# A second mixture of experts that takes its tokens in the order of the first one's slots

## The chip, the core and the metric

The kernel runs on one core of a Trainium2 chip. The core has TensorE (PE in the profile, its weight loads PEld), VectorE (DVE), ScalarE (ACT), GpSimd (POOL) and SyncE (SP), which only issues transfers here. The metric is the device time of one execution in microseconds, the median of several runs.

## The reference

Attention with pooled queries (2 batches, 8 heads, 1152 keys, 576 queries, 64 features) gives 1152 tokens of 512 features. Two mixtures of 8 experts each (hidden size 1024) follow. The first sends each token to one expert and drops what exceeds a capacity of 288 slots:

```python
expert_idx = np.argmax(x @ w_gate, axis=1)
gate_w = probs[np.arange(N), expert_idx]            # softmax of the logits
for i in range(N):                                  # slots in the order of tokens
    e = expert_idx[i]
    if counts[e] < capacity:
        disp[e, counts[e]] = x[i]; pos[i] = counts[e]; counts[e] += 1; keep[i] = True
h = np.maximum(np.einsum('ecd,edf->ecf', disp, w1), 0.0)
y = np.einsum('ecf,efd->ecd', h, w2)
out[i] = gate_w[i] * y[expert_idx[i], pos[i]]       # where keep[i], else 0
```

The second lets every expert work on every token and adds them with weights P, which come from the exponential of the logits (less their overall maximum) by eight rounds of scaling its rows and its columns:

```python
for e in range(E):
    out += P[:, e:e + 1] * (np.maximum(x @ w1[e], 0.0) @ w2[e])
```

P needs sums over all tokens, but no order of them. A dropped token enters the second mixture as zeros.

## The kernel before

Each engine has its own program, written out by hand, and they meet in semaphores. There is no scheduler: an engine does its instructions in the order of its program, and a queue its transfers in the order of issue. Products are done in three passes of split numbers (a high part, and a residue that is the value less the high part): `L1240` hidden products, `L1253` and `L1272` output products. ScalarE makes the high parts from PSUM, VectorE the residues; for weights ScalarE makes the high parts (`L512`), POOL the residues (`L448`, `L453`).

Attention: 16 heads (`head` on each engine), each of five tiles of queries. In tile t, TensorE turns the probabilities of tile t (`L1107`) and makes the scores of tile t+2 (`L1097`), into four buffers `prob`; in tile 3 it also turns out the head before (`L1140`). POOL's `split_head(g)` splits the keys, queries and values of a head that SP has loaded, L424 first and L440 last. Ahead of head 4's loads SP fills `slots_in` with zeros (L338), and one row of `slots_out` (L340).

Routing: each batch of eight heads is routed by itself, the first within heads 9 to 11, the second behind head 15. VectorE finds the best expert (L820 to L834), TensorE counts with triangular ones (`prefix`), VectorE makes the slot `sidx` (L840 to L854) and, for the way back, `gidx` (L859 to L862), and POOL scatters the rows of `x` to `slots_in` by `sidx` (L461). The gate's weight is worked out last (L908 to L922).

First mixture (`expert1`): ScalarE loads an expert's 288 rows from `slots_in`, TensorE turns them in four chunks of 128 features (`turn_rows`, L1228) within the expert before. Eight blocks of hidden products go through four PSUM banks, then four groups of 24 output products (`project_t`, L1272), one per chunk of 128 features, leave the results transposed: features on partitions, tokens along columns. ScalarE copies each (L633), TensorE turns it back into rows (`turn_back`, L1285), VectorE copies it out (L941), ScalarE stores the rows to `slots_out`. Experts 1 to 6 are a loop at run time on every engine.

Between the mixtures: POOL gathers the rows of each tile of tokens by `gidx` (L496), VectorE multiplies them by the gate (L972), TensorE turns them (`turn_tile`, L1199), ScalarE and VectorE split them into `xts`. The first three tiles come before the first hidden product, the other seven beside the next ones.

Second mixture (`expert2`): per expert three groups of 384 tokens, each of 8 x 12 hidden products and 3 x 24 output products; VectorE adds them into `acc` (L1064). The first expert also makes the logits and P (`gate_columns`, L1207, and `first_steps`). At the end ScalarE stores each tile of `acc` to the output as soon as it is done (L707).

## Time and profile before

| | |
|---|---|
| Median of 3 runs | 1359.14 us (1358.27 to 1360.24) |
| The profiled execution | 1359.23 us |
| Its span | 1357.5 us |
| Busy in the span | PE 97%, PEld 90%, DVE 39%, ACT 37%, POOL 36% |
| L1240 hidden products, both mixtures | 3072, 518.2 us busy |
| L1253, second mixture's output products | 1728, 397.7 us |
| L1272, first mixture's output products | 768, 114.1 us |
| L1285, results turned back | 96, 15.7 us |
| L1199, gathered tiles turned | 40, 7.4 us |

Busy time tells which engine is full and hardly where a change counts: matmuls are pipelined, and their ends are modelled. The chain that ended last is followed back from the last instruction, at each step to what released it; its pieces are on the path. A timeline row has start, length, engine, source line, operation, output and inputs, the number of instructions merged (x3), and in brackets the idle time of the engine ahead of it and what ended that. "issue" is time for which the profile shows no cause. SPq and ACTq rows are the issuing of transfers.

### The profile page before, as it was taken

How to read it: one execution, taken by the hardware profiler on the slowest of the kernel's cores; microseconds unless marked ns; L12 is line 12 of the kernel's file. 1: busy time of each engine (PE TensorE's matmuls, PEld its weight loads, DVE VectorE, ACT ScalarE, POOL GpSimd, SP SyncE). 2: the span in 40 equal slices, each digit the busy share in tenths (PEclk: the TensorE clock that was granted, in tenths of full speed). 3: DMA queues.
4: the chain of work that ended last, by engine and by line, in shares of the span. 5: the costliest groups of instructions: out<-in, count | busy, mean ns of one | idle time of the engine just before them, and what ended most of it. 6: DMA issues, size and time to landing. Idle time of an engine off the chain costs nothing.

```text
span 1357.5 us, 21723 instructions
## 1 busy us (share of the span) xinstructions
PE 1311.1 (97%) x7814; PEld 1225.4 (90%) x7814; DVE 522.7 (39%) x1326; ACT 505.0 (37%) x1032; POOL 488.9 (36%) x405
## 2 busy tenths in 40 slices
PE   6999999959999996999999999999999999999998
PEld 6999989949999996898999999999999999999998
DVE  7999999942222222326311112211112211112211
ACT  6777777745554553212212212212212213113111
POOL 6555556348775777102303203203203203204100
PEclk9999999979999998999999999999999999999999
DMA  4722223137666555201201201201101101100001
GB/s 134 228 96 101 97 77 112 52 135 243 205 207 189 161 183 176 89 1 32 94 0 32 93 0 52 72 0 62 62 0 62 62 0 62 62 0 0 0 0 70
DMA packets 60861, 111.95 MB, mean 82 GB/s; under 512 B 5215, under 2 KB 15779, under 8 KB 60808
## 3 DMA queue, kind: packets, MB, share of 16 engines
q1 hardware_dynamic: 52488, 94.63, 21.4%
q10 hardware_dynamic: 6848, 12.09, 2.7%
q0 software_dynamic: 1472, 4.54, 1.0%
q8 instruction: 31, 0.51, 0.2%
q14 instruction: 22, 0.18, 0.0%
HBM read 97.27 MB, written 14.16 MB: 82 GB/s over the span
## 4 chain that ended last, share of the span: by engine, by line
PE 92%; DVE 4%; issue 2%; DMA 1%; ACT 1%; POOL 0%; ACTq 0%; DVEq 0%; POOLq 0%
PE psum L1240 37%; PE psum L1253 29%; PE psum L1272 7%; PE psum L1097 6%; PE psum L1107 5%; PE psum L1122 5%; PE psum L1140 1%; PE psum L1285 1%; PE psum L1228 1%; DVE small L723 1%; DVE acts L732 1%; DVE raw L723 1%; DMA raw<-in_k_dram 0%; PE psum L1207 0%; ACT wsplit L512 0%
## 5 line engine op out<-in xcount | busy, mean ns | idle before, releaser
L1240 PE MATMUL psum<-acts,wsplit 128*128 128x384 f32 (+1 forms) x3072 | 518.2, 328 | 1.5 <-issue 1.5
L1240 PEld LDWEIGHTS psum<-acts,wsplit 128*128 128x128 f32 x3072 | 508.3, 190 | 3.8 <-issue 2.0
L1253 PE MATMUL psum<-wsplit,acts 128*128 128x512 f32 x1728 | 397.7, 390 | 0.0
L1253 PEld LDWEIGHTS psum<-wsplit,acts 128*128 128x128 f32 x1728 | 323.7, 188 | 66.3
L448 POOL TENSOR_TENSOR wsplit<-raw,wsplit 128x512 fp32r<-128x512 f32 x128 | 162.5, 1296 | 497.7 <-ACT wsplit L512 497.7
L626 ACT ACTIVATE acts<-psum 128x384 fp32r<-128x384 f32 (+1 forms) x256 | 120.7, 471 | 570.9 <-PE psum L1240 570.3
L932 DVE SCALAR_TENSOR_TENSOR acts<-psum,acts 128x384 fp32r<-128x384 f32 (+1 forms) x256 | 136.1, 532 | 374.9 <-ACT acts L626 374.7
L453 POOL TENSOR_TENSOR wsplit<-raw,wsplit 128x512 fp32r<-128x512 f32 x128 | 161.1, 1297 | 130.2 <-ACT wsplit L512 130.1
L512 ACT ACTIVATE wsplit<-raw 128x512 fp32r<-128x512 f32 (+1 forms) x259 | 155.7, 623 | 87.1 <-PE psum L1253 75.2
L1064 DVE SCALAR_TENSOR_TENSOR x<-psum,pr,x 128x512 f32<-128x512 f32 x63 | 47.3, 751 | 293.5 <-PE psum L1253 293.5
L512 ACT ACTIVATE acts<-psum 128x384 fp32r<-128x384 f32 (+2 forms) x282 | 117.1, 457 | 75.1 <-PE psum L1107 46.2
L732 DVE TENSOR_TENSOR acts<-psum,acts 128x384 fp32r<-128x384 f32 (+1 forms) x240 | 122.1, 510 | 7.0 <-ACT acts L512 6.4
L1272 PE MATMUL psum<-acts,wsplit 128*128 128x288 f32 x768 | 114.1, 300 | 0.0
L1097 PE MATMUL psum<-wsplit,acts 128*128 128x384 f32 x480 | 105.7, 356 | 7.4 <-DVE acts L873 7.4
L1272 PEld LDWEIGHTS psum<-acts,wsplit 128*128 128x128 f32 x768 | 103.1, 188 | 0.0
L1122 PE MATMUL psum<-acts,wsplit 128*128 128x256 f32 (+1 forms) x576 | 90.4, 297 | 0.6 <-ACT small L535 0.6
L1097 PEld LDWEIGHTS psum<-wsplit,acts 128*128 128x128 f32 x480 | 82.2, 193 | 7.5 <-issue 7.4
L1122 PEld LDWEIGHTS psum<-acts,wsplit 128*128 128x128 f32 x576 | 83.3, 188 | 0.7 <-DVE acts L732 0.7
L424 POOL TENSOR_TENSOR small<-small 128x576 f32<-128x576 f32 x15 | 21.3, 1419 | 94.2 <-PE psum L1097 74.5
L1107 PE MATMUL psum<-ident,small 128*128 128x128 f32 x360 | 49.1, 275 | 5.5 <-DVE acts L732 4.4
L519 ACT ACTIVATE small<-small,low 128x1152 f32<-128x1152 f32 x40 | 50.5, 1261 | 2.1 <-DVE small L723 2.1
L1107 PE MATMUL psum<-ident,raw 128*128 128x128 f32 x360 | 49.4, 278 | 1.8 <-DVE acts L732 1.4
(128 smaller groups left out, 728.3 us busy)
## 6 DMA issues: line engine op xcount, KB each, us to landing
raw<-in_moe_w_dram SPq DMA_DIRECT2D x64, 1024.0 KB, 5.1
raw<-in_k_dram SPq DMA_DIRECT2D x15, 576.0 KB, 5.9
small<-in_q_dram SPq DMA_DIRECT2D x15, 576.0 KB, 3.9
small<-in_v_dram SPq DMA_DIRECT2D x16, 288.0 KB, 4.3
slots_in<-zero SPq DMA_DIRECT2D x1, 4608.0 KB
small<-slots_in ACTq DMA_DIRECT2D x7, 576.0 KB, 4.7
slots_out<-small ACTq DMA_DIRECT2D x7, 576.0 KB, 7.1
out_dram<-x ACTq DMA_DIRECT2D x9, 256.0 KB, 2.4
```

The costliest lines, as they stand in the source:

```text
L448: pool.tensor_tensor(w1s[1][:, :, fs], raw1[hf][:, :, rsl], w1s[0][:, :, fs].bitcast(F32), ALU.subtract).then_inc(lo_done, 1)
L453: pool.tensor_tensor(w2s[1][:, f, :], raw2[f // (FC // 2)][:, f % (FC // 2), :], w2s[0][:, f, :].bitcast(F32), ALU.subtract).then_inc(lo_d ...
L512: nc.scalar.activation(out, in_, ACT.Copy).then_inc(s, 1)
L626: nc.scalar.activation(hs[0][:, f, 0:w], psum[:, f % HBANKS, 0:w], ACT.Relu).then_inc(h_hi, 1)
L732: nc.vector.tensor_tensor(pts[r][1][:, js, col:col + qw(t)], psum[:, BPT + m % TBANKS, 0:CH].rearrange("p (j n) -> p j n", j=JC)[:, :, 0:q ...
L932: nc.vector.scalar_tensor_tensor(hs[1][:, f, 0:w], psum[:, f % HBANKS, 0:w], 0.0, hs[0][:, f, 0:w].bitcast(F32), ALU.max, ALU.subtract).th ...
L1097: last = mm(psum[:, s_bank(t, c), 0:CH], qs[u][i][:, t * P:(t + 1) * P], ksp[u][:, c * CH:(c + 1) * CH], start=(i == 0), stop=(i == 1))
L1107: last = nc.tensor.transpose(psum[:, BPT + m % TBANKS, j * P:(j + 1) * P], prob[buf(v, t)][:, (c * JC + j) * P:(c * JC + j + 1) * P], iden ...
L1122: last = mm(psum[:, BPV, 0:GW[r]], vsp[v % 2][:, j, :], pts[r][i][:, j, :], start=(n == 0), stop=(n == VSTEPS - 1))
L1240: last = mm(psum[:, f % HBANKS, 0:w], w1s[a][:, c, f * P:(f + 1) * P], src[z][:, c, cols], start=(i == 0), stop=(i == 3 * DC - 1))
L1253: last = mm(psum[:, bank, :], hs[a][:, f, t0:t0 + P], w2s[z][:, f, :], start=(i == 0), stop=(i == 3 * FC - 1))
L1272: last = mm(psum[:, BY + c % 2, 0:CAP], w2s[a][:, f, c * P:(c + 1) * P], hs[z][:, f, 0:CAP], start=(i == 0), stop=(i == 3 * FC - 1))
```

## The change

The results of the first mixture stay on the chip, transposed as they come, and the second mixture takes the tokens in the order of experts and slots instead of their own.

- The gate's weight multiplies the rows before they are scattered. It is positive, and the maximum with zero keeps it. VectorE works it out within the routing (`gate_input`, `gate_weight`); rows of batch 0 are scaled by POOL in heads 11 to 13, those of batch 1 by ScalarE (two tiles) and VectorE (three).
- TensorE adds up how many tokens each expert has (`totals`), VectorE makes of it at which column each expert's tokens start (`expert_starts`), and the token's place (`owner_index`). POOL scatters each token's number to `owners` by it, within experts 0 to 3.
- `y_cols` on ScalarE and VectorE splits the four groups of an expert's results straight into `xts`, from the starting column on, which each engine reads into a register once per expert (`value_load`). Columns behind an expert's last token are written over by the next expert; ScalarE clears those past the last (`clear_x`).
- The first four hidden blocks of the second mixture begin with three of their four chunks of features.
- SP clears the output ahead of head 4's loads, since dropped tokens have no owner; POOL scatters the tiles of `acc` to the output by `owner`.
- For room: three probability buffers, values in another place, `xts` 288 columns wider, `dts` apart from it. The experts of the first mixture are written out on all engines, in place of a loop.

The diff, cut:

```diff
-        NP = 4
+        NP = 3
...
+            sp.dma_start(out.rearrange("(p a) (b c) -> p (a b) c", p=P, c=P),
+                         zero[:, :].unsqueeze(1).broadcast_to([P, NT * DC, P])).then_inc(out_cleared, 16)
+            sp.wait_ge(consts, 20)
+            sp.dma_start(owners.rearrange("(p a) o -> p (a o)", p=P), nobody[:, :]).then_inc(owners_cleared, 16)
...
+            def scale_early(t):
+                pool.wait_ge(x_done, NH)
+                pool.wait_ge(gate_done, 1)
+                part = x[0:qw(t), t, 0:DM]
+                pool.tensor_tensor(part, part, gate[0:qw(t), t:t + 1].broadcast_to([qw(t), DM]),
+                                   ALU.mult).then_inc(scaled0, 1)
...
+            def own(n):
+                w = qw(n % QT)
+                pool.indirect_dma_start(
+                    out=owners, out_offset=bass.IndirectOffsetOnAxis(ap=cidx[0:w, n:n + 1], axis=0),
+                    in_=token[0:w, n:n + 1], in_offset=None,
+                    bounds_check=N - 1, oob_is_err=False).then_inc(owned, 16)
...
+                if n == 1:
+                    pool.wait_ge(cidx_done, 1)
+                    pool.wait_ge(owners_cleared, 16)
+                for m in OWN.get(n, ()):
+                    own(m)
...
+            pool.wait_ge(owner_loaded, 16)
+            pool.wait_ge(out_cleared, 16)
+            for n in range(NT):
+                pool.wait_ge(y_done, NT * (E - 1) + n + 1)
+                pool.indirect_dma_start(
+                    out=out, out_offset=bass.IndirectOffsetOnAxis(ap=owner[:, n:n + 1], axis=0),
+                    in_=acc[:, n, :], in_offset=None,
...
+            def y_cols(e, start_e, c):
+                if e:
+                    act.wait_ge(yx_done, DC * (e - 1) + c + 1)
+                split_hi(xts[0][:, c, bass.ds(start_e, CAP)], psum[:, BY + (DC * e + c) % 3, 0:CAP], yx_hi)
...
+                if e == 0:
+                    act.wait_ge(starts_ready, 1)
+                start_e = act.value_load(starts[0:1, e:e + 1], min_val=0, max_val=min(e * CAP, N))
+                if e:
+                    act.wait_ge(x_cleared, 2 * min(e, N // CAP - 1))
...
+            def gate_weight(b):
+                ts = tiles(b)
+                dve.wait_ge(ex_done, b + 1)
+                rstep(nc.vector.tensor_reduce(sume[:, ts], ex[:, ts, :], AXX, ALU.add))
+                rstep(nc.vector.tensor_scalar_add(sume[:, ts], sume[:, ts], EPS))
+                nc.vector.reciprocal(gate[:, ts], sume[:, ts]).then_inc(gate_done, 1)
...
             one_hot(1)
+            gate_input(1)
             scale_output(G - 1)
+            gate_weight(1)
             slot_limit(1)
             slot_number(1)
             scatter_index(1)
...
+            for t in range(ACT_ROWS, QT):
+                scale_rows(t)
+            expert_starts()
+            owner_index()
...
+            def y_cols(e, start_e, c):
+                if c == 0 and e:
+                    dve.wait_ge(x_cleared, 2 * min(e, N // CAP - 1))
+                dve.wait_ge(yx_hi, DC * e + c + 1)
+                cols = bass.ds(start_e, CAP)
+                nc.vector.tensor_tensor(xts[1][:, c, cols], psum[:, BY + (DC * e + c) % 3, 0:CAP],
+                                        xts[0][:, c, cols].bitcast(F32), ALU.subtract).then_inc(yx_done, 1)
...
+                if DC * e + c >= 3:
+                    pe.wait_ge(yx_done, DC * e + c - 2)
...
+                    opening = HBANKS if first and g == 0 else 0
+                    for f in range(opening):
+                        pe.wait_ge(h_done, FC * E + f - HBANKS + 1)
+                        hidden(E, f, xts, cols, TG, range(DC - 1), yx_done if f == 0 else None, DC * (E - 1))
+                    for f in range(opening):
+                        hidden(E, f, xts, cols, TG, range(DC - 1, DC), yx_done if f == 0 else None, DC * (E - 1))
+                    for f in range(opening, FC):
+                        pe.wait_ge(h_done, FC * E + NG * FC * e + FC * g + f - HBANKS + 1)
+                        hidden(E + e, f, xts, cols, TG, range(DC), None, 0)
```

In the instructions TensorE's stream changes at the seam of the mixtures. Before, from the middle of the last expert's last output group on (L1285 turns results back, L1199 turns gathered tokens, L1240 is the second mixture's first hidden block):

```order
L1272 MATMUL psum<-acts,wsplit 128x288 x12
L1285 MATMUL psum<-ident,small 96x128 [waits y_done,yt_done]
L1285 MATMUL psum<-ident,small 96x128 x2
L1199 MATMUL psum<-ident,x 128x128 [waits x2_scaled]
L1199 MATMUL psum<-ident,x 128x128 x3
L1199 MATMUL psum<-ident,x 128x128 [waits x2_scaled]
L1199 MATMUL psum<-ident,x 128x128 x3
L1199 MATMUL psum<-ident,x 128x128 [waits x2_scaled]
L1199 MATMUL psum<-ident,x 128x128 x3
L1240 MATMUL psum<-acts,wsplit 128x384 [waits lo_done,xt_done,h_done]
L1240 MATMUL psum<-acts,wsplit 128x384 x11
```

and afterwards (L1311 is the output group, L1279 a hidden block):

```order
L1311 MATMUL psum<-acts,wsplit 128x288 [waits yx_done]
L1311 MATMUL psum<-acts,wsplit 128x288 x23
L1279 MATMUL psum<-acts,wsplit 128x384 [waits yx_done,lo_done,h_done]
L1279 MATMUL psum<-acts,wsplit 128x384 x2
L1279 MATMUL psum<-acts,wsplit 128x384 [waits yx_done]
L1279 MATMUL psum<-acts,wsplit 128x384 x2
L1279 MATMUL psum<-acts,wsplit 128x384 [waits yx_done]
L1279 MATMUL psum<-acts,wsplit 128x384 x2
L1279 MATMUL psum<-acts,wsplit 128x384 [waits lo_done,h_done]
L1279 MATMUL psum<-acts,wsplit 128x384 x8
L1279 MATMUL psum<-acts,wsplit 128x384 [waits lo_done,h_done]
L1279 MATMUL psum<-acts,wsplit 128x384 x8
```

The transposes are gone, and so is the wait for gathered rows; the last chunk's columns are waited for only where the fourth chunk begins, further on.

VectorE behind the choice of the second batch's experts, before (`oh` marks the expert, `sidx` is the slot):

```order
L834 TENSOR_TENSOR oh<-eqr,st 128x40 [waits route_step]
L761 TENSOR_TENSOR x<-psum,den 128x5x64
L840 TENSOR_TENSOR cnt<-elim,oh 128x40 [waits oh_done]
L841 TENSOR_REDUCE st<-cnt 128x5 [waits route_step]
L847 TENSOR_TENSOR cnt<-psum,oh 128x40 [waits pos_ready,route_step]
L849 TENSOR_REDUCE st<-cnt 128x5 [waits pos_read]
L853 TENSOR_TENSOR st<-st 128x5 [waits route_step]
L854 SCALAR_TENSOR_TENSOR sidx<-st 128x5 [waits route_step]
L859 SCALAR_TENSOR_TENSOR st<-st 128x5
L861 TENSOR_SCALAR st<-st 128x5 [waits route_step]
L862 CAST gidx<-st 128x5 [waits route_step]
```

and afterwards (L906 is the exponential's input, L911 to L913 the gate's weight in `st`, L887 the limit):

```order
L882 TENSOR_TENSOR oh<-eqr,st 128x40 [waits route_step]
L906 TENSOR_TENSOR tmp<-lg,st 128x40
L810 TENSOR_TENSOR x<-psum,den 128x5x64
L911 TENSOR_REDUCE st<-ex 128x5 [waits ex_done]
L912 TENSOR_SCALAR st<-st 128x5 [waits route_step]
L913 RECIPROCAL st<-st 128x5 [waits route_step]
L887 TENSOR_SCALAR st<-st 128x5
L894 TENSOR_TENSOR cnt<-psum,oh 128x40 [waits pos_ready,route_step]
L896 TENSOR_REDUCE st<-cnt 128x5 [waits pos_read]
L900 TENSOR_TENSOR st<-st 128x5 [waits route_step]
L901 SCALAR_TENSOR_TENSOR sidx<-st 128x5 [waits route_step]
L920 TENSOR_SCALAR x<-x,st 128x512 [waits x_done,gate_done]
```

Three operations of the gate now stand ahead of the slot, one more ahead of the scaling of the output, and the three for `gidx` are gone.

ScalarE in an expert of the loop, where its hidden evacuations end, before (L621 and L630 prepare the waits of the loop, L512 writing `acts` splits turned tokens, L633 takes a result):

```order
L512 ACTIVATE wsplit<-raw 128x4x128
L625 REGISTER_ALU
L626 ACTIVATE acts<-psum 128x288 [waits h_ready]
L512 ACTIVATE wsplit<-raw 128x4x128
L621 REGISTER_ALU
L512 ACTIVATE acts<-psum 128x288 [waits dt_ready]
L621 REGISTER_ALU
L512 ACTIVATE acts<-psum 128x288 [waits dt_ready]
L630 REGISTER_ALU
L632 REGISTER_ALU [waits y_ready]
L633 ACTIVATE small<-psum 128x288 [waits rows_ready]
```

and afterwards (L713 reads the register; L564 writing `acts` with `yx_done` splits a result):

```order
L686 ACTIVATE acts<-psum 128x288 [waits h_ready]
L564 ACTIVATE wsplit<-raw 128x4x128
L713 TENSOR_LOAD starts
L713 ISA x2
L564 ACTIVATE acts<-psum 128x288 [waits dt_ready,x_cleared]
L564 ACTIVATE acts<-psum 128x288 [waits dt_ready]
L564 ISA [waits yx_done,y_ready]
L564 ACTIVATE acts<-psum 128x288
```

The register load stands between the last weight split and the first turned tokens of the next expert.

## Rows read from the trace of the kernel before

**Rows 1.** Page, chain that ended last: shares of the span by engine.

```profile
PE 92%; DVE 4%; issue 2%; DMA 1%; ACT 1%; POOL 0%; ACTq 0%; DVEq 0%; POOLq 0%
```

**Rows 2.** Chain, one expert of mixture one: start us, us, what it consists of.

```profile
361.18 1.58 PE psum L1240 x12
...
380.02 0.33 PE psum L1285 x3
...
389.17 1.59 PE psum L1240 x12
```

**Rows 3.** Timeline, TensorE between the mixtures: start us, us, engine line op out<-in xcount [idle<-releaser].

```profile
526.16 1.82 PE L1272 MATMUL psum<-acts,wsplit 128*128 128x288 f32 x12
...
537.23 1.12 PE L1199 MATMUL psum<-ident,x 128*128 128x128 f32 x4 [7.61 <-DVE x L972]
...
542.57 4.18 PE L1240 MATMUL psum<-acts,wsplit 128*128 128x384 f32 x12 [1.46 <-issue]
```

**Rows 4.** Chain, second mixture, first and a steady stretch.

```profile
565.81 5.48 PE psum L1253 x24
...
660.47 16.66 PE psum L1240 x96
```

**Rows 5.** Timeline between the mixtures, ScalarE's last result and POOL's first gather.

```profile
528.65 0.39 ACT L633 ACTIVATE small<-psum 128x288 f32<-128x288 f32 x1
...
533.10 1.07 POOL L496 DMA_INDIRECT x<-slots_out,gidx  x1 [1.20 <-DMA slots_out<-small]
```

**Rows 6.** Timeline, routing of the second batch.

```profile
287.80 0.19 DVE L840 TENSOR_TENSOR cnt<-elim,oh 128x40 f32<-128x40 f32 x1
...
288.91 0.17 DVE L854 SCALAR_TENSOR_TENSOR sidx<-st 128x5 uint32<-128x5 f32 x1
...
289.88 1.01 POOL L461 DMA_INDIRECT slots_in<-x,sidx  x1 [31.46 <-DVE gidx L862]
...
290.04 0.23 DVE L920 TENSOR_REDUCE st<-ex 128x10 f32<-128x80 f32 x1 [0.34 <-ACT ex L604]
```

**Rows 7.** Chain, the scatter of the second batch.

```profile
293.74 0.97 POOL slots_in L461
...
295.02 2.31 DMA slots_in<-x,sidx
```

**Rows 8.** Timeline, where an expert's hidden products end: ScalarE and TensorE's weight loads.

```profile
374.62 0.62 ACT L512 ACTIVATE wsplit<-raw 128x512 fp32r<-128x512 f32 x1
...
376.09 0.28 PEld L1228 LDWEIGHTS psum<-ident,small 96*128 96x128 f32 x3 [0.18 <-DVE acts L926]
```

**Rows 9.** Timelines of SP, POOL and TensorE around heads 4 and 5.

```profile
35.94 15.63 SPq L340 DMA_DIRECT2D slots_out<-zero  x1
...
59.38 1.41 POOL L424 TENSOR_TENSOR small<-small 128x576 f32<-128x576 f32 x1 [10.64 <-DMA small<-in_q_dram]
...
67.52 1.41 POOL L440 TENSOR_TENSOR acts<-small,acts 128x576 fp32r<-128x576 f32 x1
...
75.34 1.29 PE L1097 MATMUL psum<-wsplit,acts 128*128 128x384 f32 x6
...
91.79 0.42 PE L1097 MATMUL psum<-wsplit,acts 128*128 128x384 f32 x1
```

**Rows 10.** Windows: length, busy PE, PEld, DVE, ACT, POOL, clock, DMA share, GB/s.

```profile
40.00:44.00 4.00, 4.00 (x34) 3.97 (x34) 3.94 (x11) 2.56 (x6) 3.83 (x4) 1.00 1.12 334
232.00:248.00 16.00, 15.93 (x120) 15.49 (x119) 15.21 (x48) 12.52 (x28) 9.67 (x9) 1.00 0.21 65
```

**Rows 11.** Timeline of head 9, POOL beside VectorE.

```profile
181.26 1.42 POOL L440 TENSOR_TENSOR acts<-small,acts 128x576 fp32r<-128x576 f32 x1
...
181.63 1.11 DVE L840 TENSOR_TENSOR cnt<-elim,oh 128x40 f32<-128x40 f32 x1
```

**Rows 12.** Timeline, POOL's w2 residues, with the idle time ahead.

```profile
386.83 6.31 POOL L453 TENSOR_TENSOR wsplit<-raw,wsplit 128x512 fp32r<-128x512 f32 x5 [7.93 <-ACT wsplit L512]
```

**Rows 13.** Timeline, VectorE's last accumulation.

```profile
1354.27 0.75 DVE L1064 SCALAR_TENSOR_TENSOR x<-psum,pr,x 128x512 f32<-128x512 f32 x1 [4.68 <-PE psum L1253]
```

433 lines of the change are left out of this document (194 added, 239 removed).

## The prediction, made before the changed kernel ran

> **What bounds the kernel now.** I read the shares of the chain that ended last first, then the chain row by row where the change acts, then the timelines around those places. The chain lies on TensorE for 92% of the span [rows 1]: what counts is how many microseconds TensorE multiplies, transposes or waits. Three places matter.
>
> In the first mixture an expert takes 28.0 us (361.18 to 389.17) [rows 2]. In it stand the products, the transposes of the next expert's tokens, and four transposes of finished results back into rows, each 0.33 us on the chain [rows 2].
>
> Between the mixtures TensorE's last product starts at 526.16 and twelve products of 288 columns take 1.6 (0.134 us each, the 12 behind 361.18 take 1.58), so it ends at 527.75 [rows 2, 3]. The first transpose of gathered tokens follows at 537.23, the first hidden product at 542.57 [rows 3], and the first output product at 565.81 [rows 4]. POOL's first gather starts only at 533.10, after the stored rows have landed [rows 5]. In the steady state the 96 hidden products between those two points take 16.66 [rows 4].
>
> Behind the attention, the routing of the second batch goes through a string of short VectorE operations that ends at 289.08, then POOL scatters [rows 6]; nothing else runs on TensorE there.
>
> **What the change takes away.**
> 1. Transposes back. Experts 0 to 7 have 4 each; the last of expert 7 stands behind the final product, and expert 0 has three within its stream, as the rest of its four stands in expert 1. That makes 31 within the stream, 31 x 0.33 = 10.2 us, all on the chain. The copies and stores that followed them lay beside products. The work put in their place is one ScalarE and one VectorE operation per 128 features, as before, and the output ring of three banks instead of two lets TensorE do two further groups of 24 products (3.2 us each) before it must wait for either. Term: -10.2.
> 2. The hand-over. From the last product to the first output product of the second mixture it is 565.81 - 527.75 = 38.1 us. Afterwards the 96 hidden products follow at once: 16.7. Its cover: the first 36 of them (four banks, three of the four feature chunks) take 36 x 0.174 = 6.2 us, until 534.0 on the old scale, and need nothing of the last chunk. ScalarE took up that last chunk at 528.65 [rows 5] behind seven weight splits, and VectorE follows within about 1 us: 4 us to spare. The banks come free in time too: the four are finished 0.52 apart, bank 0 is asked for again 1.56 after its end, and its two evacuations take about 1. Term: 38.1 - 16.7 = -21.4.
>
> **What it adds or moves.**
> 3. The gate in the routing. The weight must be in the rows before they are scattered. Order on VectorE: one operation ahead of the scaling of the output, three behind it, and one less for the limit. The sum behind the exponential waited 0.34 for ScalarE [rows 6]; the output's scaling, which now stands between, covers that. Three linked operations of 0.17 to 0.23 and one of 0.2, less one of 0.2: sidx comes 0.7 later than 289.08. Scaling two tiles on ScalarE and three on VectorE (at most 0.62 each, as a weight split [rows 8]) lies beside POOL, whose scatters stand 1.28 apart [rows 7]. ScalarE's weight splits now begin behind it, at some 290.2; 12 of at most 0.62 end at 297.6, ahead of the scatter's landing at 297.3 + 0.7 [rows 7]. Past that each would delay the load of the rows. Term: +0.7 (bounds 0.2 and 1.5).
> 4. Clearing the output. 4608 more pieces of 512 B (2.36 MB) stand in SP's queue right in front of head 4's keys and queries. SP sat 15.63 us at the small copy behind the 4.72 MB zero fill before it gave out head 4's loads; POOL began its split of them at 59.38, after waiting 10.64 for the queries, and its last operation ended at 68.93. TensorE's scores of head 4 began at 75.34: 6.4 us of slack. The queues carried 334 GB/s then, of which the fill is about 305 (4.72 MB in 15.5): 2.36 MB are 7.7 us [rows 9, 10]. Head 4 is ready at 76.6, 1.3 late. Head 5's queries, asked for when POOL is done, land some 4 us later, and POOL's 9.55 us of work ends near 90.3, before TensorE asks for it (91.79 + 1.3). VectorE is busy 3.94 of 4 us there [rows 10], so nothing wins this back. Term: +1.3 (bounds 0 and 3: below if only part of the fill's time goes ahead of the load, above if head 5 is caught as well).
> 5. Reading the expert's first column. On ScalarE a register load stands between the last hidden evacuation with its weight split and the evacuation of the next expert's first turned tokens; TensorE waits for the latter already, 0.18 us each time [rows 8]. The trace has no such load. Lower bound 0: the weight split before it starts at 374.62 and takes 0.62, and a load given out beside it is hidden. Upper bound 1.3: the distance from one POOL scatter to the next, the only instructions here that read an index in memory [rows 7]. I take 0.3, near the lower end since 0.5 of the engine's own time can hide it; seven experts have a successor: +2.1 (bounds 0 and 9.1). VectorE's load hides the same way.
> 6. Heads 9 to 13. VectorE loses 1.11 at 181.63 for an operation that takes 0.19 at 287.80 when POOL is still [rows 6, 11]. A single-operand form replaces it in the same place, four short operations are added in heads 9 and 10, three leave head 11, and POOL scales five tiles (1.3 each, by its splits of the same size [rows 12]) in heads 11 to 13, where VectorE's reciprocals run. Added and removed nearly balance. Term: +0.5 (bounds -1 and 2).
> 7. The end. The last accumulation ends at 1355.02, and with ScalarE's store the span of 1357.5 ends 2.5 later [rows 13]. POOL instead starts 0.8 to 0.9 after its release (289.08 to 289.88, [rows 6]) and its scatter lands 2.3 after the start [rows 7]. Term: +0.8 (bounds -0.2 and 1.9).
> 8. At nothing: three probability buffers (the wait for the third-last tile's turning is implied by TensorE's own order of scores), the other place of the values, clearing of columns on ScalarE (1152 elements, 1.4 by the 0.62 of 512, twice in three experts; a step of 1.6 us uses some 1.0 of it, and there are four banks), the owners' scatters (three of 1.3 in POOL's idle 7.93 before the w2 residues [rows 12]; uncovered they would be 13 us of weights), their load, and the straight-line experts.
>
> **Two rules weighed.** Rows 8 show what follows the place of the register load, not the load. The Trainium skill, Runtime: NRT & Kernel Launch, under Instruction fetch mechanics, has about 200 ns per register for such a load, and under The ~15µs preamble/postamble breakdown 1.3 us for several words from HBM. As an estimate, the first makes seven loads 1.4 and hidden, the second 9.1 and mostly seen. No run here shows it for SBUF.
>
> Rows 11 show VectorE's 1.11 ending (182.74) as POOL's operation ends (182.68). The Trainium skill, SBUF — State Buffer, under Who interferes with whom, says that a VectorE operation with two SBUF inputs and a GpSimd operation that reads SBUF shut each other out for a whole instruction. By that rule, the trace agrees, POOL's new scaling speaks against the change: up to 1.3 per head for three heads, the upper bound of step 6 and more.
>
> **The sum.** 1359.23 - 10.2 - 21.4 + 0.7 + 1.3 + 2.1 + 0.5 + 0.8 = 1333.0 us. The profiled execution's 1359.23 (span 1357.5 and 1.7 around it) lies 0.1 above the median of the runs, so this stands for the median too.
>
> **The rivals.**
> A. The register load waits until ScalarE is drained. For: it must follow its engine's order, and TensorE waits at that spot already. Against: 0.5 of cover. Price 1.3 x 7 = 9.1 in place of 2.1: 1340.0.
> B. The attention gives back more: head 5 caught too, POOL's scaling in VectorE's way in three heads. For: VectorE is busy 15.21 of 16 us. Against: POOL is busy 9.67 of 16 [rows 10]. Price 1.7 (step 4's upper bound) + 1.5 (step 6's) + 2 beyond it: about 1338.
> C. Steps 4 to 6 are hidden. For: 6.4 of slack and 0.5 of cover are of the order of the costs. Price -3.9: 1329.1.
> D. Slower: the first mixture's experts, now straight code with twice the instructions before the second mixture, starve TensorE of instructions. It decides from (26.2 + 2.7) / 8 = 3.6 us per expert on; at 4 us each the time is 1333.0 + 32 = 1365. Against: the heads are straight code already, and the two windows of rows 10 show TensorE busy 4.00 of 4 and 15.93 of 16 us.
> E. The change does not do what it says: the second mixture still waits, since the last chunk comes behind the weight splits. From 4 us lateness on; to keep even 10 of the 21.4 (time 1343) the last chunk would need to be 14 late. Against: rows 5.
>
> **Chances.** Forecast 0.55 (1330 to 1336.5), A 0.16, B 0.1, C 0.14, D 0.02, E 0.03. The range to hold 8 in 10 takes in C and most of A and B: 1328 to 1341. Differences under 0.2% (2.7 us) can't be told from none here; faster 0.97, the same 0.01, slower 0.02: only D ends there.
>
> **What would show it.** Steps 1 and 2: no transposes but those of tokens in an expert, about 26.7 us plus the load's share per expert, and the output product of the second mixture some 17 us behind the last of the first, with no idle TensorE between. Step 4: head 4's scores wait about 1.3 for POOL. Step 5: TensorE's wait before the second transpose of an expert, 0.18 now, is 0.5; at 1.5 it is A. Step 3: the first scatter 0.7 later against the end of the attention. Step 7: 3.2 from the last accumulation to the end. Wrong would be an expert over 28 us, an idle TensorE between the mixtures, or a gap above 3 us at head 4 or 5.

## The result, and the profile after

| | before | after |
|---|---|---|
| median of 4 runs each, us | 1359.69 (1358.27 to 1362.77) | 1341.51 (1340.81 to 1342.95) |
| ratio, 95% interval | | 0.987 (0.9858 to 0.9883) |
| profiled execution, span | 1359.23, 1357.5 | 1340.81, 1339.1 |
| TensorE busy | 1311.1 | 1296.7 |

The changed kernel is faster by 1.3%. The forecast was 1333.0, with 1341 as the range's end: the direction and the large terms were right, but 7.8 us of the 26.2 forecast did not come, and the result lies outside the range. Spans divided at the same events show where:

| stretch | before | after | difference | forecast |
|---|---|---|---|---|
| start to turning out head 15 | 284.45 | 289.39 | +4.9 | +1.8 (steps 4, 6) |
| to the second batch's first scatter | 5.43 | 5.76 | +0.3 | +0.7 (step 3) |
| to expert 0's first hidden product | 13.11 | 13.31 | +0.2 | 0 |
| to the end of mixture one's last product | 224.76 | 217.36 | -7.4 | -8.1 (steps 1, 5) |
| to mixture two's first output product | 38.06 | 16.85 | -21.2 | -21.4 (step 2) |
| to TensorE's end | 788.24 | 790.65 | +2.4 | 0 |
| to the end of the span | 3.45 | 5.78 | +2.3 | +0.8 (step 7) |

The page's chain by engine answers to [rows 1]: still TensorE, one point less.

```profile
PE 91%; DVE 3%; issue 1%; ACT 1%; DMA 1%; POOL 1%; POOLq 0%; DVEq 0%; ACTq 0%
```

The chain through one expert of mixture one (start us, us, what), against [rows 2]: 365.72 to 392.62 is 26.90 in place of the 27.99 between 361.18 and 389.17, and no transpose is left but those of tokens (L1268). The issue of 0.03 at 380.39 is all that shows where the register load stands. In [rows 8] the second transpose's weight load waited 0.18.

```profile
365.72 12.80 PE psum L1279 x96
378.52 0.25 PE psum L1268 x3
378.76 1.62 PE psum L1311 x12
380.39 0.03 issue
380.42 0.44 PE psum L1268 x3
...
382.73 3.23 PE psum L1311 x24
...
392.62 2.40 PE psum L1279 x18
```

The chain between the mixtures, against [rows 3, 4]: the hidden products follow the last output products with no gap, and at 542.67 the first output products follow them.

```profile
513.02 12.80 PE psum L1311 x96
525.82 16.84 PE psum L1279 x96
```

The steady stretch of mixture two, against [rows 4]: 96 hidden products take 16.84 where they took 16.66, and nothing waits.

```profile
653.23 16.34 PE psum L1292 x72
669.57 16.84 PE psum L1279 x96
```

The timelines of the queue of SyncE, of POOL and of TensorE at heads 3 and 4, against [rows 9] (three cuts of three timelines). SyncE gives out head 4's keys at 59.64 (before: 51.61), behind two clearings that hold its queue. POOL starts on them 8.3 late. What TensorE lacks is not head 4's scores, as forecast, but the values of head 3, which POOL splits in the same round (L441, ends at 75.11): it idles 4.42.

```profile
35.75 16.38 SPq L357 DMA_DIRECT2D out_dram<-zero  x1
52.17 7.42 SPq L360 DMA_DIRECT2D owners<-nobody  x1
59.64 1.20 SPq L320 DMA_DIRECT2D raw<-in_k_dram  x1
...
67.72 1.43 POOL L453 TENSOR_TENSOR small<-small 128x576 f32<-128x576 f32 x1 [19.82 <-DMA small<-in_q_dram]
...
73.71 1.40 POOL L441 TENSOR_TENSOR wsplit<-raw,wsplit 128x576 fp32r<-128x576 f32 x1
...
69.49 1.29 PE L1139 MATMUL psum<-wsplit,acts 128*128 128x384 f32 x6
75.21 2.05 PE L1164 MATMUL psum<-acts,wsplit 128*128 128x256 f32 x8 [4.42 <-issue]
77.05 2.12 PE L1149 MATMUL psum<-ident,small 128*128 128x128 f32 x9
...
80.89 1.27 PE L1182 MATMUL psum<-raw,small 128*128 128x72 f32 x10
```

The same two points before, the product with head 3's values and the turning out of head 2, which stands in head 3:

```profile
73.28 1.10 PE L1122 MATMUL psum<-acts,wsplit 128*128 128x256 f32 x8
...
76.47 1.23 PE L1140 MATMUL psum<-raw,small 128*128 128x72 f32 x10
```

Behind the gap everything is slow: nine transposes in 2.12, where nine took 1.14 at 68.59. The windows (columns as in [rows 10]) show why: behind the idle time the granted clock is at 0.50, 1.2 in place of 2.4 GHz.

```profile
70.00:75.00 5.00, 0.79 (x5) 0.47 (x3) 2.80 (x9) 1.67 (x4) 4.75 (x4) 0.91 0.00 0
75.00:78.00 3.00, 2.79 (x13) 2.82 (x14) 0.00 (x0) 0.07 (x1) 2.13 (x3) 0.50 0.00 0
78.00:82.00 4.00, 4.00 (x23) 4.00 (x21) 2.61 (x8) 2.64 (x5) 0.66 (x1) 0.63 0.95 303
```

The chain in expert 0: it comes from the landing of late weights, and TensorE stands idle for 1.19 ahead of the second transposes (row with e8 below).

```profile
311.09 10.30 DMA raw<-in_moe_w_dram
```

The end, against [rows 13]: the timeline's last addition ends at 1334.30, the scatter's record starts at 1335.09 and the span ends at 1339.1.

```profile
1333.54 0.75 DVE L1106 SCALAR_TENSOR_TENSOR x<-psum,pr,x 128x512 f32<-128x512 f32 x1 [4.68 <-PE psum L1292]
1335.09 0.97 POOL L555 DMA_INDIRECT out_dram<-x,owner  x1 [4.46 <-DVE x L1106]
```

### The profile page after: what moved, and what is told of

The parts are those of the page before. It is cut to its first block, busy times and chain, and to the rows that moved or that the text cites. A ratio compares the mean times of both kernels' runs of the same rounds, so it can differ in the third digit from the quotient of the medians.

```text
span 1339.1 us, 20887 instructions
## 1 busy us (share of the span) xinstructions
PE 1296.7 (97%) x7688; PEld 1213.4 (91%) x7688; DVE 508.0 (38%) x1313; ACT 505.7 (38%) x1031; POOL 502.9 (38%) x423
## 4 chain that ended last, share of the span: by engine, by line
PE 91%; DVE 3%; issue 1%; ACT 1%; DMA 1%; POOL 1%; POOLq 0%; DVEq 0%; ACTq 0%
PE psum L1279 36%; PE psum L1292 29%; PE psum L1311 8%; PE psum L1149 6%; PE psum L1139 5%; PE psum L1164 5%; PE psum L1182 1%; DMA raw<-in_moe_w_dram 1%; POOL wsplit L479 1%; DVE raw L772 1%; PE psum L1268 1%; DVE acts L781 1%; DVE small L772 0%; ACT acts L564 0%; ACT raw L571 0%
## 5 line engine op out<-in xcount | busy, mean ns | idle before, releaser
L1279 PE MATMUL psum<-acts,wsplit 128*128 128x384 f32 (+1 forms) x3072 | 515.4, 328 | 0.0
L1279 PEld LDWEIGHTS psum<-acts,wsplit 128*128 128x128 f32 x3072 | 509.3, 189 | 1.8
L564 ACT ACTIVATE wsplit<-raw 128x512 fp32r<-128x512 f32 (+1 forms) x259 | 155.3, 623 | 85.2 <-PE psum L1292 75.0
L564 ACT ACTIVATE acts<-psum 128x384 fp32r<-128x384 f32 (+2 forms) x304 | 123.1, 448 | 121.4 <-PE psum L1311 55.5
L1311 PE MATMUL psum<-acts,wsplit 128*128 128x288 f32 x768 | 109.2, 298 | 0.0
L1311 PEld LDWEIGHTS psum<-acts,wsplit 128*128 128x128 f32 x768 | 103.2, 188 | 0.0
L1149 PE MATMUL psum<-ident,raw 128*128 128x128 f32 x477 | 64.4, 275 | 4.1 <-ACT raw L571 2.2
L571 ACT ACTIVATE raw<-raw,low 128x1152 f32<-128x1152 f32 x53 | 66.9, 1262 | 0.0
L772 DVE TENSOR_SCALAR_CACHE_REDUCE raw<-psum,low 128x384 f32<-128x384 f32 x106 | 64.4, 607 | 0.1
L1149 PEld LDWEIGHTS psum<-ident,raw 128*128 128x128 f32 x477 | 52.7, 140 | 10.6 <-ACT raw L571 5.2
```

The lines of the kernel that those rows point to most:

```text
L564: nc.scalar.activation(out, in_, ACT.Copy).then_inc(s, 1)
L1149: last = nc.tensor.transpose(psum[:, BPT + m % TBANKS, j * P:(j + 1) * P], prob[buf(v, t)][:, (c * JC + j) * P:(c * JC + j + 1) * P], iden ...
L1279: last = mm(psum[:, f % HBANKS, 0:w], w1s[a][:, c, f * P:(f + 1) * P], src[z][:, c, cols], start=(c == 0 and (a, z) == (0, 0)), stop=(c == ...
L1311: last = mm(psum[:, BY + (DC * e + c) % 3, 0:CAP], w2s[a][:, f, c * P:(c + 1) * P], hd[z][:, f, :], start=(i == 0), stop=(i == 3 * FC - 1))
```

## The experiments

All are edits of the changed kernel (1341.5, ratio 0.987) but e4, an edit of the kernel before. Ratios are to the kernel before as it ran beside each group of them (medians 1358.4 to 1360.2 us), with 95% intervals. A single letter is the theory of that name in the expectation above it. Code is cut, with "..." for what is left out.

| | median, us | ratio |
|---|---|---|
| e1_pitch1408 | 1336.84 | 0.9831 (0.9811 to 0.9851) |
| e2_late_clear | 1334.95 | 0.9831 (0.9812 to 0.985) |
| e3_vector_clears | 1351.4 | 0.9944 (0.9927 to 0.996) |
| e4_before_odd | 1363.25 | 1.0031 (1.002 to 1.0042) |
| e5_shift | 1336.94 | 0.9837 (0.9824 to 0.9851) |
| e6_fixed_starts | 1340.03 | 0.9858 (0.9843 to 0.9873) |
| e7_direct_store | 1338.36 | 0.9837 (0.9824 to 0.9851) |
| e8_clears_later | 1340.27 | 0.9855 (0.9838 to 0.9872) |
| e9_owners_late | 1341.15 | 0.9855 (0.984 to 0.987) |
| e10_no_opening | 1343.13 | 0.9874 (0.9859 to 0.989) |
| e11_pitches | 1335.8 | 0.9825 (0.9811 to 0.9838) |
| e12_all | 1329.5 | 0.9769 (0.9756 to 0.9783) |
| e13_pitch1344 | 1337.59 | 0.9841 (0.9816 to 0.9866) |
| e14_hold | 1343.99 | 0.9892 (0.9874 to 0.991) |

### The fill: e2 and e9

e2 issues the output's clearing far later, behind the loads of the second mixture's first expert, and the owners' behind those of head 6:

```diff
-sp.dma_start(out..., zero...).then_inc(out_cleared, 16)      # ahead of head 4
+sp.dma_start(out..., zero...).then_inc(out_cleared, 16)      # behind load_expert(1, 0, E)
```

> The changed kernel with the clearing of the output moved in SP's queue from ahead of head 4's loads to behind the loads of the second mixture's first expert, and the small clearing of owners to behind head 6's loads. Theory F (fill): the fill alone held head 4's queries back 8.3 us, TensorE idled 4.4 at head 3 and then ran some 5 us at half the granted clock, and head 4 lost 1.1 to a POOL that was shifted. The turning-out behind head 15 then goes from 289.39 to about 283.1, time 1335.2. Rival G (gate work): POOL's scaling of rows and the gate's operations in heads 9 to 13 take part of the 4.9; then it stays above 285. Rival H: with the fill away the old stall at head 2 (2.1 us, VectorE's 1.8 us operation beside POOL) returns in full on top: time 1337.

Head 15 was turned out at 283.45, 5.9 earlier, and the time fell by 6.6: F. In its timeline POOL starts on head 4 at 58.97 and TensorE has no gap at the values of head 3. H's old stall did come back (TensorE idles 0.93 and 0.55 for VectorE ahead of 68.12, where the kernel before idled 0.90 and 0.55), within the 5.9 and not on top of them. G is out: 283.45 is under its 285, and ahead of the kernel before.

```profile
35.73 16.47 SPq L320 DMA_DIRECT2D raw<-in_k_dram  x1
...
72.87 1.11 PE L1165 MATMUL psum<-acts,wsplit 128*128 128x256 f32 x8
```

e9 tells which clearing is to blame; it moves the owners' alone.

> Only the filling of the small table of owners (7.42 us in SyncE's queue in the changed kernel, 52.17 to 59.59) goes behind head 6's loads; the clearing of the output stays ahead of head 4. Head 4's keys are then issued at 52.2 and not at 59.64 (before: 51.61). O, the owners' table is what makes head 4 late: no 4.42-us wait of TensorE at head 3, turning out behind head 15 begins at 283.5 to 284.5 and not at 289.39, time about 1336. Q, the 16 us of clearing ahead of it keep the loads late by filling the DMA engines, wherever the table's issue stands: 288 to 289, 1341.

```profile
35.57 16.27 SPq L357 DMA_DIRECT2D out_dram<-zero  x1
51.89 7.55 SPq L320 DMA_DIRECT2D raw<-in_k_dram  x1
...
74.74 1.61 PE L1165 MATMUL psum<-acts,wsplit 128*128 128x256 f32 x8 [4.31 <-issue]
```

The 7.5 us simply went over to head 4's keys, which now stand in that place, and head 15 was turned out at 287.84: Q, though not quite as written. The row's time is not that of its own transfer. Whatever stands first behind the 4.7-MB fill sits 15.6 to 16.5 us in SyncE's queue (slots_out of 2 KB before, the output's clearing after, the keys in e2), and what stands behind the 2.4-MB clearing sits 7.4 to 7.6. A small DMA carries the wait for its predecessors in the profile.

### The distance between rows: e1, e4, e5, e13, e11

The change made a row chunk of xts 1440 columns (5760 B) long in place of 1152 (4608 B). e1 takes 1408 (5632 B), e4 gives the kernel before 1184 (4736 B), with hd at 288 and dts at 384.

```diff
-        XW = N + CAP
+        XW = 1408
```

> The changed kernel with one difference: a chunk of the second mixture's tokens (xts) lies 1408 columns behind the last instead of 1440, 5632 B = 11 x 512 B instead of 5760 B = 22.5 x 256 B. Theory P (pitch): TensorE reads its moving columns more slowly where a chunk does not begin on a round address; the 96 hidden products of the second mixture go back from 16.84 us to the 16.66 of the kernel before, in 24 groups: 24 x 0.18 = 4.3 us, time 1337.2. Rival L (load): the 0.18 comes from what else changed around them (clock, other engines at SBUF); 16.84 stays, time 1341.5.

> The kernel before with three pitches changed and nothing else: xts 1184 columns (4736 B, no multiple of 256) in place of 1152, the first mixture's hidden values 288 columns in place of 384, its turned tokens 384 in place of 288. Theory P: three separate readings: hidden products of the second mixture 16.66 -> 16.84 per 96, output products of the first 3.16 -> 3.21 per 24, hidden products of the first 12.80 -> 12.65 per 96; in sum 4.3 + 1.6 - 1.1 = +4.8 us, time 1364. Rival L: all three as before, 1359.4.

Both fit P. e4 shows its other two readings as well: in mixture one 96 hidden products take 1.58 + 11.06 = 12.64, where the kernel before took 1.58 + 11.19, and an expert's output products some 0.1 more. From the chains, e1 first, then e4, each in the steady stretch of mixture two:

```profile
669.94 16.66 PE psum L1279 x96
```

```profile
660.14 16.84 PE psum L1244 x96
```

From mixture two's first hidden product to the last scatter e1 takes 2.6 us less (1332.25 - 525.38 against 1335.09 - 525.66), not the 24 x 0.18 = 4.3 of the hidden products: the output products take 16.36 for 16.34, and in e1 the clock dropped once more, in the gate's steps (12 products in 3.16 for 2.31, the next 24 in 4.77 for 4.22; see the last section). e5 shifts both halves by 256 B at distance 1408:

> Row distance of xts 1408 columns as in e1, but both halves begin 64 columns (256 B) further on, so that every stretch that the hidden products read begins 256 B off the place it had. In e1 96 hidden products took 16.66 us, in the changed kernel (where chunks 1 and 3 of 4 lie 256 B off and 0 and 2 do not) 16.84. P, the distance between the rows is what counts: 16.66 us, and 806.9 us from the first hidden product of mixture two to the last scatter, as in e1 (about 1337). A, the place of each read counts, and half of them are misplaced in the changed kernel: all are now, 16.66 + 2 x 0.18 = 17.02 us, 24 groups make 8.6 us more, 815.5 (about 1346).

It has 16.66 too (at 667.62), so A is out: not where a stretch begins but how far apart the rows are. e13 tells which distances:

> Row distance of xts 1344 columns, 5376 B: a multiple of 256 B (21) and not of 512 B (10.5). The slow distances so far (5760, 4736 and 1152 B) are multiples of neither, the fast ones (4608, 5632 and 1536 B) of both. H, whole 512 B are needed: 96 hidden products of mixture two in 16.84 us, about 1341. Q, whole 256 B do: 16.66 us, about 1338.

```profile
669.44 16.66 PE psum L1279 x96
```

Q: 5376 B, 21 x 256, is fast. All fast distances tried are whole multiples of 256 B, the slow ones are not. e11 gives hd and dts whole multiples as well (1536 B for 1152):

```diff
-        XW = N + CAP
-        HD = 2 * FC * CAP
+        XW = 1152
+        HD = 2 * FC * TG
...
-        hd = [acts[...FC * CAP...] ...]
+        hd = [hs[i][:, :, 0:CAP] for i in (0, 1)]
+        dts = ... DC * TG ... [:, :, 0:CAP]
```

> All operands that TensorE reads as columns lie in rows whose distance is a multiple of 512 B: xts 1152 columns (4608 B; these inputs' slots end at column 1114), hd and dts 384 (1536 B). R, the distance is what made the products slower: 96 hidden products of mixture two 16.66 us for 16.84 (24 groups, less 0.02 for each of 24 output groups: 2.4 us in all as measured with 1408), the period of an expert 26.90 less 0.24 (output products 12 in 1.58 for 1.61) and less 0.14 (hidden products 96 in 12.66 for 12.80, as with the distance 384 in the kernel before): 8 x 0.38 = 3.0 us; 1336.1. V, only xts matters: 1339.1.

R, but less than its 3.0 us: the expert's period is 26.64 (the chain below), so 8 x 0.26 = 2.1. The hidden products are as expected (12.64), the output products of mixture one went only from 3.23 to 3.19 per 24. The hidden part was not lost by the change: dts lay at 1152 B in the kernel before too. The change moved hd alone in mixture one, from 1536 B to 1152.

```profile
363.71 12.64 PE psum L1279 x96
...
380.56 3.19 PE psum L1311 x24
...
390.35 9.74 PE psum L1279 x74
```

### The clears of slots: e3 and e8

e3 lets VectorE make the clears of columns, with the same shape:

```diff
-                nc.scalar.activation(xts[i][:, :, k * CAP:(k + 1) * CAP], zero..., ACT.Copy)
+                nc.vector.tensor_copy(xts[i][:, :, k * CAP:(k + 1) * CAP], zero...)
```

> The changed kernel with the six clearings of columns done by VectorE instead of ScalarE, at the same places. Theory C (clears): in expert 0 ScalarE comes late to the first turned tokens because of two clearings of 1.17 us, and TensorE waits 1.19 us for them; without them the wait is about 0.2, time 1340.4. Rival W (weights): ScalarE is late there because expert 1's first weights land late (it waits 4.39 and 0.66 for them in expert 0); the wait stays at 1 or more and the time at 1341.5.

All theories missed: 10 us slower than the changed kernel. The timelines of VectorE, POOL and TensorE in expert 0:

```profile
318.38 12.30 DVE L1003 CAST acts<-zero 128x1152 fp32r<-128x1152 f32 x1
...
331.34 0.80 DVE L1003 CAST acts<-zero 128x1152 fp32r<-128x1152 f32 x1
...
320.16 9.90 POOL L479 TENSOR_TENSOR wsplit<-raw,wsplit 128x512 fp32r<-128x512 f32 x8
...
333.37 0.71 PE L1267 MATMUL psum<-ident,x 96*128 96x96 f32 x3 [9.12 <-DVE acts L984]
```

A copy that takes 0.80 when POOL splits nothing took 12.30 and ended at 330.68, 0.6 us behind POOL's row of splits (330.06). ScalarE's clear of the same shape takes 1.17 beside the same splits. It is the effect that [rows 11] show at 1.11 for 0.19, but here VectorE did not get in between POOL's operations and waited for the rest of the row, about nine of them. That is one of the six clears. The other four that ran beside such a row, in experts 1 and 2, took 1.44, 1.28, 1.44 and 1.27, and they did get in between: POOL's own split beside them took 1.83 for 1.3.

```profile
354.77 1.44 DVE L1003 CAST acts<-zero 128x1152 fp32r<-128x1152 f32 x1
...
355.54 1.83 POOL L479 TENSOR_TENSOR wsplit<-raw,wsplit 128x512 fp32r<-128x512 f32 x1
```

What made the first one wait so long stays open. The Trainium skill, SBUF — State Buffer, under Who interferes with whom, has copies and casts of VectorE that use both port pairs shut out GpSimd and be shut out by it for whole instructions, and ScalarE wait for no one; by that page this was the engine not to move the clears to, and the trace agrees. In expert 0 TensorE idled 9.12, 7.9 more than in the changed kernel, and behind it the granted clock was at 0.50 (window 333:336); together that is most of the 10 us.

e8 moves expert 0's two clears by ScalarE into expert 1. It does one thing more than its expectation says: the clears that experts 1 and 2 have of their own come one step later (`f in (4, 6)` in place of `(3, 5)`).

> The two clears of slots that ScalarE makes in expert 0 (1.17 and 1.15 us) are made in expert 1 in front of its own two, where ScalarE is idle half of the time; nothing else moves. S, the clears are what makes ScalarE late in expert 0: the one behind the last late weight (322.76) lies on the chain, the first lies in a wait for that weight, so 1.05 us of the 1.19 us in front of L1268 go, 1340.4. W, the late weights alone do it: 1.19 us stay, 1341.5. B, four clears in expert 1 hold up the hidden splits: a new wait of TensorE there of up to 2 us, 1343.

The profiled span is that of the changed kernel, 1339.1. The timelines of ScalarE, VectorE and TensorE in expert 0, the changed kernel first:

```profile
321.42 0.63 ACT L564 ACTIVATE wsplit<-raw 128x512 fp32r<-128x512 f32 x1 [0.66 <-DMA raw<-in_moe_w_dram]
...
326.60 0.44 PE L1268 MATMUL psum<-ident,x 96*128 96x96 f32 x3 [1.19 <-DVE acts L991]
```

```profile
322.32 0.63 ACT L564 ACTIVATE wsplit<-raw 128x512 fp32r<-128x512 f32 x1 [2.22 <-DMA raw<-in_moe_w_dram]
...
325.85 0.46 DVE L993 TENSOR_TENSOR acts<-psum,acts 128x288 fp32r<-128x288 f32 x1 [0.46 <-ACT acts L564]
...
326.46 0.44 PE L1270 MATMUL psum<-ident,x 96*128 96x96 f32 x3 [0.81 <-POOL wsplit L479]
```

From the split of the late weight to the second transposes it is 5.18 in the changed kernel and 4.14 in e8. The other runs repeat it: 5.15 to 5.19 in the ten that leave ScalarE's clears where they were, 4.13 in e12, which moves them. So 1.04 us of expert 0's wait are the second clear's, which stands behind that split, as S has it. They did not show in full in e8's wait, 0.81 for 1.19, because the weight itself landed 0.9 later there. POOL, which the profile names as what ended the wait, is a coincidence: the transposes wait for VectorE's residue (`dt_done`), which ended at 326.31, and POOL's operation ended at 326.36.

What e8 gained it gave back in experts 1 and 2. There the later clear holds the next transposes, 0.33 of idle TensorE each where 0.03 to 0.05 stood. In expert 2, whose chain follows, that can only come from the shift of its own clears, since none of expert 0's stands there.

```profile
378.01 0.96 ACT acts L696
...
380.82 0.44 PE psum L1270 x3
```

With the clears in place the wait in expert 0 is anything from 0.47 (e6) to 1.81 (e1), mostly according to when that weight lands against TensorE's products.

### The register load: e6

```diff
-                start_e = act.value_load(starts[0:1, e:e + 1], ...)
+                start_e = min(144 * e, N - CAP)
```

The kernel leaves out the experts' own first columns, so its output is not the reference's.

> The experts' first columns are constants, 144 x e, and nothing is loaded into registers; the second mixture's columns are then not the experts' own slots, and its output is not the reference's. T, the trace of the changed kernel is right that the load costs 0.06 us in each of 7 experts: 0.4 us less, 1341.1, the expert's period stays 26.90 less 0.06, and the 0.24 us in front of L1268 becomes 0.18. P, the prediction's 0.3 us an expert: 2.1 us less, 1339.4. A, the register load drains its queue: 9 us less, 1332.4.

The time fell by 1.5, and the ratios' intervals overlap. The trace is clearer: hidden blocks start at 417.66 and 444.58, a period of 26.92 as with the load (419.52 and 446.41: 26.89), and the place of the load shows 0.05 of issue (378.49). What this execution gained lies in the fill (288.35) and in expert 0's wait. The load costs nothing that can be seen, less even than T's 0.06; P and A are out.

### The end: e7

```diff
-                pool.indirect_dma_start(out=out, out_offset=...owner..., in_=acc[:, n, :], ...)
+                act.dma_start(out[n * P:(n + 1) * P, :], acc[:, n, :])
```

The kernel leaves out the way back to the tokens' own rows.

> The ten output tiles are stored by ScalarE's direct DMAs in the order of slots in place of GpSimd's scatter by owner, so the output's rows are not in the reference's order. In the changed kernel the last scatter is issued at 1335.09 behind 0.51 + 1.19 us of queue on GpSimd and the span ends 4.0 us later, 4.76 us behind the last addition (1334.33); before, the span ended 3.45 us behind TensorE's last product, now 5.78. E, the indirect scatter is what makes the end longer: 2.3 us less, 1339.2. N, a direct store's landing takes as long: 1.7 us of queue less at most on GpSimd and as much back on ScalarE, 1341 or more.

```profile
1334.14 0.75 DVE L1105 SCALAR_TENSOR_TENSOR x<-psum,pr,x 128x512 f32<-128x512 f32 x1 [4.68 <-PE psum L1291]
1334.92 0.34 ACTq L756 DMA_DIRECT2D out_dram<-x  x1
```

The span ends at 1337.3, 2.4 behind the addition's end (1334.89), for 4.8 with the scatter: E.

### The hand-over: e10 and e14

e10 drops the opening (`opening = 0`); e14, whose edit is shown, keeps it and makes its first product wait for the fourth column group.

```diff
+                    if opening:
+                        pe.wait_ge(yx_done, DC * E)
```

> The second mixture's first hidden products no longer begin with the three column groups that are ready and come back for the fourth; the first of them waits until the last expert's fourth group is split. In the changed kernel they begin at 525.82 and VectorE's last split is 527.35 + 0.46 and 0.14 to TensorE. M, the opening is what closes the hand-over without idle time: TensorE waits 2.1 us before its first product, 1343.6. N, something else (the order of the weights) holds the first products anyway: no wait, 1341.5. C, the clock falls behind the wait as it does at head 3: 2.1 us and up to 3 us more, 1346.

> TensorE waits for the last expert's fourth column group before the first hidden product of mixture two; the products keep their new order. In e10 only the fourth chunk's products waited (0.46 us), since three chunks of the first column group, 1.6 us of products, still ran ahead. M, the late group is covered by the 36 products ahead of it and by nothing else: TensorE idles 2.1 us from 525.8 on (527.35 + 0.46 + 0.14), 1343.6, and its clock stays whole. C, the clock falls behind this gap as behind the 4.42 us at head 3: 2.5 us more, 1346. N, the group is there sooner than VectorE's record shows: under 1 us, 1342.

e10's time is close to M's 1343.6, but not for M's reason. Its timeline shows 0.46 of idle and not 2.1, since nine products of the first block still ran ahead, and the granted clock stayed at 1.00 (window 528:532). From its first hidden product to the first output product it is 17.74 (525.97 to 543.71) for 16.84, so dropping the opening costs 0.9 there. The rest of the 3.0 by which its profiled execution is longer lies elsewhere: 1.5 in a clock drop in the gate's steps (568:572 at 0.67), 0.45 in a VectorE operation of the later steps, 0.15 ahead of the hand-over. e14 holds all products back, in timeline and windows:

```profile
526.52 18.66 PE L1279 MATMUL psum<-acts,wsplit 128*128 128x384 f32 x96 [2.03 <-DVE acts L1006]
```

```profile
525.00:528.00 3.00, 1.48 (x6) 1.46 (x7) 0.46 (x1) 1.35 (x4) 3.00 (x4) 0.85 0.00 0
528.00:532.00 4.00, 4.00 (x18) 4.00 (x17) 0.00 (x0) 0.00 (x0) 4.00 (x4) 0.68 0.74 256
```

M's idle time (2.03) and, behind it, C's clock: 96 products in 18.66 for 16.84. Here the wait in one piece costs 2.03 + 1.82 = 3.85 us. Its profiled execution is only 3.0 longer, since it came to this point 1.3 earlier and lost 0.45 later on. So the late group is worth 3.85 if nothing covers it, and 0.9 if the blocks merely go in their plain order: the opening itself gains the 0.9.

### Together: e12

e11's rows, e2's later clearings, and expert 0's clears made in expert 1 at its first two steps.

> The changed kernel with what the runs point to: rows as in e11 (2.4 + 3.0 us by R), both clearings issued later as in e2 (6 us), and expert 0's clears of slots made in expert 1, early enough that its last split isn't held (0.4 us, as measured with them at its end, where that gave the 0.4 us back). The sum: 1341.5 - 5.4 - 6.0 - 0.4 = 1329.7. V, only xts matters: 1332.7. I, the fill's loads and the clearing behind head 15 collide with the second weights of mixture one as they did not in e2: over 1335.

1329.5 against 1329.7 by the sum. That they meet so closely is partly chance: the sum took 3.0 for mixture one's rows, where e11's period gives 2.1, and 0.4 for the clears, where 1.04 were to be had. It beats both kernels: 12.0 us under the changed one, 2.3% under the one before. It relies on the slots of these inputs ending at column 1114.

## Why the forecast was wrong, step by step

**Step 4, the step that failed.** It put the fill at +1.3 with 3 as the bound. e2, which differs only in where the two clearings are issued, shows 5.9. The start of each turning out of a head, from the timelines:

| head turned out | before | changed | e2 |
|---|---|---|---|
| 1 | 58.37 | 57.57 | 57.54 |
| 2 (in head 3) | 76.47 | 80.89 | 76.07 |
| 3 (in head 4) | 92.92 | 98.47 | 92.54 |
| 7 | 158.74 | 164.25 | 158.34 |
| 10 | 211.60 | 216.54 | 210.65 |
| 15 | 284.45 | 289.39 | 283.45 |

Against the kernel before, heads 3 and 4 lose 5.5. The delay of the load was right (8.0 in SyncE's queue against 7.7). Three things were not:

- The waiter. The round of POOL that begins with head 4's keys also splits head 3's values, needed by the product that ran at 73.28 before. It ran at 75.21, 1.9 late, where the forecast had 1.3 for the scores.
- The clock, which the step did not have. The kernel before idled 0.90 and 0.55 between 66 and 69, because a VectorE operation had taken 1.81 beside POOL. With POOL late this did not occur (the same operation took 0.19), so TensorE ran ahead and then idled 4.42 in one piece, and the clock fell behind it. From the late product to the turning out of head 2 it took 5.68 for 3.19, 2.5 more.
- Head 4, 1.1 more, where VectorE's L794 took 1.45 beside the shifted POOL.

Of rival B only the direction came: head 5 was not caught (16.44 from head 3's turning out to head 4's, before 16.45), and POOL's scaling cost nothing that can be seen (step 6). e2 gives all 5.9 back.

**Step 6.** Forecast +0.5, bounds -1 and 2. By the table the changed kernel takes 52.29 from head 7 to head 10 where the kernel before took 52.86, and from head 10 to head 15 both take 72.85: -0.6. The kernel before has two VectorE operations held up there (L840 1.11, L853 1.35), the changed one a single one (L887 1.08). POOL's five scalings ran at 195.25, 206.86 and 223.36, 1.0 each, and no VectorE operation took over 0.8 between 195 and 272. So the up to 1.3 per head that the prediction feared of them did not come: in this trace nothing ran into them.

**Not in the forecast at all: slower products.** Row distances that are no multiples of 256 B. In mixture two 23 groups x 0.18 = 4.1, less 0.5 for the output products, less 1.3 for a clock drop that this execution was spared: the 2.4 of the table. In mixture one an expert takes 0.2 more than the kernel before without its transposes back, 1.6 in all, but the distance explains only a part: the output products of an expert take 12.86 for 12.74 (12.75 in e11), 0.12 or 1.0 in eight experts. The rest is spread over pieces of 0.05 and less. The columns' distance is a line of the diff, and the rows showed 16.66 for the old one; the step that should have asked was "at nothing" (8).

**Step 7.** Forecast +0.8, bound 1.9, found 2.3. The addition's end to the scatter's record is 0.8, as taken; the rest is 4.0 behind the record's start, where 2.3 was taken from the chain of the earlier scatter [rows 7]. e7 shows the 2.4 for a direct store. Why this scatter ends later behind its start than the earlier one stays open.

**Step 5.** Forecast +2.1 with A at 9.1; e6 shows nothing. The lower bound was the right end.

**Step 8, the clears.** Priced at nothing since ScalarE had 0.6 of a step to spare. True in the steady state, not in expert 0, where the weights land late (the chain waits for their DMA until 321.42) and no spare is left: TensorE waits 1.2, and 1.04 of it are the second clear's own, by e8 and e12.

**Right.** Step 2: 21.2 for 21.4. Its cover was there as named: VectorE's last split starts at 527.35, and the four banks' first 36 products run until 532. Step 3: +0.3, within its bounds. The owners' scatters ran in POOL's idle time as stated; its wait before the w2 residues went from 7.93 [rows 12] to 3.17. D and E did not occur.

**Right in part by luck.** Step 1: 31 x 0.33 are gone, and 1.2 (expert 0) and 1.6 (0.2 an expert) were given back, so the mixture is 7.4 shorter. That is near the 8.1 forecast only because the 2.1 priced for the register load, which did not come, stood for 2.8 that were not priced.

## What to carry to other kernels

Ask of every wait that you add how long TensorE will idle in one piece, and count the products behind it at half the clock as a possible cost: 4.4 us of idle time cost 2.5 more (head 3), 2.0 cost 1.8 (e14), and behind 0.46 (e10) the clock stayed whole. When a change alters the shape of a buffer, compare the distance between its rows before and after as you would an instruction count. When a load is late, list everything that the engine makes in the same round, and follow the first consumer, not the one by which the round is named.

## What was not expected of the hardware

- The moving operand's row distance: 96 products of 384 columns take 16.66 us at 4608, 5376 and 5632 B, 16.84 at 4736 and 5760 B; 96 of 288 columns 12.64 at 1536 B and 12.80 at 1152 B. A shift of the start by 256 B changes nothing.
- Beside POOL's splits one copy by VectorE from and to SBUF waited for the rest of the row, 12.30 us for 0.80, while four others waited for part of one operation (1.27 to 1.44).
- The clock behind TensorE's short, small products in the gate's steps fell in some executions and not in others, with the same instructions there (it fell in the kernel before, e1, e3, e7, e9, e10, e12 and e13). It costs 1.3 us and more: the same twelve hidden products take 2.38 in the changed kernel and 3.67 in e7. Windows of e7, then of the changed kernel:

```profile
568.00:570.00 2.00, 2.00 (x7) 2.00 (x7) 0.00 (x0) 0.00 (x0) 0.00 (x0) 0.50 0.00 0
```

```profile
568.00:572.00 4.00, 4.00 (x25) 3.91 (x24) 0.74 (x2) 0.49 (x1) 0.00 (x0) 1.00 0.00 0
```

What decides it stays open, and so does what makes the late weight of expert 0 land sooner or later.
